# Expert layer with a fixed room of 832 rows for each expert, its weights standing and its rows moving, and attention matmuls in halves

## What is computed

```python
for t in range(S):                                   # attention
    state = f[:, :, t, :, None] * state + np.einsum('bhd,bhe->bhde', k[:, :, t], v[:, :, t])
    y[:, :, t] = np.einsum('bhd,bhde->bhe', q[:, :, t], state)
...
noisy_logits = x @ w_gate + np.log1p(np.exp(x @ w_noise)) * noise
top2 = np.argpartition(-noisy_logits, 2, axis=1)[:, :2]
...
h = np.maximum(x[mask] @ w1[e], 0.0)                 # w1: 384 x 1024, for each of 8 experts
out[mask] += top2_w[mask, k, None] * (h @ w2[e])     # w2: 1024 x 384
...
g = h - np.tanh(h)                                   # h = x @ w_in, 384 x 2048
return g @ w_out                                     # 2048 x 384
```

## Time and profile before

| | |
|---|---|
| runs shown, median | 1233.32 us (1232.97 to 1234.04) |
| the profiled execution, its own time | 1235.88 us |
| its span, first to last instruction | 1234.0 us |
| PE busy | 1121.3 us, 91% of the span |
| DVE, ACT, POOL busy | 482.3, 371.4, 264.9 us |
| chain that ended last | PE 83%, DVE 8%, issue 3% |

### The profile page before, as it was taken

One profiled execution on the slowest core, in us unless ns is written; L12 is line 12 of the kernel. 1 busy time (PEld: TensorE's weight loads), 2 busy tenths in 40 slices (PEclk: granted clock), 3 DMA queues, 4 the chain that ended last, 5 costly groups with the idle time before them and its releaser, 6 DMA issues.

```text
span 1234.0 us, 17874 instructions
## 1 busy us (share of the span) xinstructions
PE 1121.3 (91%) x6761; PEld 1011.8 (82%) x6762; DVE 482.3 (39%) x946; ACT 371.4 (30%) x707; POOL 264.9 (21%) x167
## 2 busy tenths in 40 slices
PE   4999796806999999999999999759999999999999
PEld 3888685805999999989998999649999999999998
DVE  3777574743222222222222222254343433434333
ACT  3444332321222222222222222323233332333322
POOL 1001203064242504224051433032010111100000
PEclk9999787957999999999999999969999999999999
DMA  8213213154323221314141414021020101110000
GB/s 330 70 67 99 94 59 134 48 202 172 141 63 117 96 89 54 132 39 145 42 143 38 147 38 147 31 71 52 1 65 13 52 26 42 37 39 13 21 6 26
DMA packets 34271, 98.71 MB, mean 80 GB/s; under 512 B 4784, under 2 KB 23344, under 8 KB 31152
## 3 DMA queue, kind: packets, MB, share of 16 engines
q0 software_dynamic: 9024, 50.34, 11.9%
q1 hardware_dynamic: 17136, 36.71, 9.0%
q10 hardware_dynamic: 8064, 11.01, 2.4%
HBM read 70.71 MB, written 27.33 MB: 79 GB/s over the span
## 4 chain that ended last, share of the span: by engine, by line
PE 83%; DVE 8%; issue 3%; DMA 2%; another core or an unknown queue 2%; ACT 1%; DVEq 0%; SPq 0%; POOL 0%; ACTq 0%
PE bank L762 18%; PE bank L754 18%; PE bank L852 16%; PE bank L864 16%; PE bank L775 4%; PE bank L650 2%; PE bank L674 2%; PE bank L768 1%; DMA noise_sb<-noise 1%; PE bank L671 1%; DVE kT L938 1%; DVE state L967 1%; PE bank L626 1%; PE bank L658 1%
## 5 line engine op out<-in xcount | busy, mean ns | idle before, releaser
L864 PE MATMUL bank<-slots,g_hi 128*128 128x384 f32 x768 | 196.5, 336 | 0.0
L754 PE MATMUL bank<-slots,x_hi 128*128 128x512 f32 x624 | 166.6, 403 | 2.8 <-issue 1.5
L762 PE MATMUL bank<-slots,h_hi 128*128 128x384 f32 x832 | 159.9, 344 | 2.6 <-DVE h_lo L1229 2.6
L852 PE MATMUL bank<-dx_hi,slots 128*128 128x512 f32 x576 | 152.4, 400 | 1.3 <-DVE dx_lo L1262 1.3
L864 PEld LDWEIGHTS bank<-slots,g_hi 128*128 128x128 f32 x768 | 141.2, 188 | 8.2
L762 PEld LDWEIGHTS bank<-slots,h_hi 128*128 128x128 f32 x832 | 144.8, 190 | 2.9 <-issue 2.9
L754 PEld LDWEIGHTS bank<-slots,x_hi 128*128 128x128 f32 x624 | 114.9, 191 | 26.7 <-issue 4.0
L864 PE MATMUL bank<-slots,g_lo 128*128 128x384 f32 x384 | 129.6, 337 | 0.0
L852 PEld LDWEIGHTS bank<-dx_hi,slots 128*128 128x128 f32 x576 | 106.8, 190 | 19.1 <-issue 1.6
L517 ACT ACTIVATE h_hi<-bank 128x512 fp32r<-128x512 f32 x104 | 56.5, 595 | 203.8 <-PE bank L775 203.8
L1271 DVE TENSOR_TENSOR g_lo<-g,g_hi 128x512 fp32r<-128x512 f32 x96 | 66.5, 692 | 121.2 <-ACT g_hi L574 121.2
(11 more groups left out here) (151 smaller groups left out, 1456.2 us busy)
## 6 DMA issues: line engine op xcount, KB each, us to landing
raw_w<-w_all POOLq DMA_DIRECT2D x20, 1536.0 KB, 7.0
qkv_sb<-qkv SPq DMA_DIRECT2D x24, 576.0 KB, 3.7
xg<-expert_rows SPq DMA_DIRECT2D x53, 192.0 KB, 2.3
expert_outs<-y_sb ACTq DMA_DIRECT2D x52, 192.0 KB, 1.9
f_exp<-f SPq DMA_DIRECT2D x4, 1152.0 KB, 17.8
out<-d_out SPq DMA_DIRECT2D x24, 192.0 KB, 2.0
expert_outs<-zeros SPq DMA_DIRECT2D x7, 192.0 KB
expert_rows<-zeros ACTq DMA_DIRECT2D x4, 192.0 KB, 1.9
```

The lines of the kernel that those rows point to most:

```text
L754: done = mm(ps[:, :], x_part[:, k, :], slots[:, base + at:base + at + BANK], start=n == 0 and k == 0, stop=n == 2 and k == DK - 1)
L762: done = mm(pO[:, 0:D], h_part[:, k, :], slots[:, base + at:base + at + D], start=start and n == 0 and k == 0, stop=stop and n == 2 and k ...
L852: done = mm(pDH[s % 2][:, :], slots[:, at:at + P], x_part[:, b % 2, k, :], start=n == 0 and k == 0, stop=n == 2 and k == DK - 1)
L864: done = mm(pD[j][:, 0:D], g_part[:, s % 2, j * P:(j + 1) * P], slots[:, at:at + D], start=c == 0 and n == 0, stop=c == FC - 1 and n == 2)
```

## The change

1. Every expert has a fixed room of `CAP` = 832 rows in `expert_rows`, and results lie at the same place in `expert_outs`. The table `meta` and `out_row_a/b` go away; a block behind `If(overflowing(...))` on each engine handles rows beyond 832, and does not run with the inputs here.
2. The expert layer takes the form of the dense one: 16 parts (448 and 384 rows of each expert), 8 steps of 128 hidden columns each, all written out. Weights are stationary and rows move on the way up (9 matmuls of 448 or 384 columns); on the way down there are 4 or 3 tiles, each 3 matmuls of 384 columns. Nothing is transposed between them. Copies of results go half to ACT, half to DVE, and SP stores them.
3. The whole room is filled with zeros at the start, by 8 DMAs of 832 rows (10.2 MB together) that ACT issues ahead of its first activation; the first scatter waits for them (`zeroed`).
4. The matmuls with the state, with `am` and of the gate scores are cut into two halves of 64 output rows, twice as many as before.
5. `route_rows` has two operations more; rows of the dense layer are split one step later (`c - 1 in X_STEPS`).

```diff
+PIECES = (448, 384)
+CAP = sum(PIECES)
...
+HALVES = (slice(0, P // 2), slice(P // 2, P))
...
             sp.wait_ge(scattered, 2 * NT * 16)
             sp.wait_ge(early_done, 1)
+            load_rows(0)
+            load_rows(1)
+            for i in range(len(PARTS)):
+                if i + 2 < len(PARTS):
+                    sp.wait_ge(m_xT_ps, M_FIRST[i + 1])
+                    load_rows(i + 2)
+                store_rows(i)
...
+            pool.wait_ge(zeroed, -(-CLEARED // CAP) * 16)
             for g in range(B):
                 scatter(g, g)
...
+            act.wait_ge(zeros_ready, 1)
+            for row in range(0, CLEARED, CAP):
+                some = expert_rows[row:min(row + CAP, CLEARED), :].rearrange("(p j) d -> p j d", p=P // 2)
+                act.dma_start(some, zeros[0:P // 2, :].unsqueeze(1).to_broadcast(list(some.shape))).then_inc(zeroed, 16)
             act.wait_ge(L_zeroed, 1)
             decay_exp(0, f_in[0], 16)
...
+            for s in range(M_STEPS):
+                i, c = divmod(s, FK)
+                m_h_high(s)
+                if i + 1 < len(PARTS) and 1 <= c <= M_TILES[i + 1]:
+                    m_x_high(i + 1, c - 1)
+                if i >= 1 and c == 1:
+                    m_results(i - 1)
+            m_results(len(PARTS) - 1)
...
-                    done = mm(pG[:, D:D + GATES], xT32[:, k * P:(k + 1) * P], wr[:, k, :],
-                              start=k == 0, stop=k == DK - 1)
+                    for half in HALVES:
+                        cols = slice(k * P + half.start, k * P + half.stop)
+                        done = mm(pG[half, D:D + GATES], xT32[:, cols], wr[:, k, :],
+                                  start=k == 0, stop=k == DK - 1)
...
-                    mm(pY[:, c0:c0 + 2 * HD], qT[:, a, :], state[:, a, :, :].rearrange("p c d -> p (c d)"),
-                       start=True, stop=False, skip_group_check=True)
+                    for half in HALVES:
+                        mm(pY[half, c0:c0 + 2 * HD], qT[:, a, half], state[:, a, :, :].rearrange("p c d -> p (c d)"),
+                           start=True, stop=False, skip_group_check=True)
...
+            def m_up_chunk(s):
+                i, c = divmod(s, FK)
+                e, off, n = PARTS[i]
+                if c == 0:
+                    pe.wait_ge(m_xlo, M_FIRST[i + 1])
+                    if off == 0:
+                        pe.wait_ge(w_split, 2 * (e + 1))
+                if s >= 2:
+                    pe.wait_ge(m_hlo, s - 1)
+                for q, (lo, x_part) in enumerate(up_terms):
+                    for k in range(DK):
+                        at = e % 2 * SLOT + lo * PART + k * F + c * P
+                        done = mm(pDH[s % 2][:, 0:n], slots[:, at:at + P], x_part[:, i % 2, k, 0:n],
+                                  start=q == 0 and k == 0, stop=q == 2 and k == DK - 1)
+                done.then_inc(m_up, 1)
+
+            def m_down_chunk(s):
+                i, c = divmod(s, FK)
+                e, off, n = PARTS[i]
+                pe.wait_ge(m_hlo, s + 1)
+                for j in range(M_TILES[i]):
+                    if c == 0 and i >= 1 and j < M_TILES[i - 1]:
+                        pe.wait_ge((m_y_act, m_y_dve)[j % 2], y_done(i - 1, j))
+                    first = part_out(n, j)
+                    for q, (g_part, lo) in enumerate(((g_hi, 0), (g_hi, 1), (g_lo, 0))):
+                        at = e % 2 * SLOT + lo * PART + WCOLS + c * D
+                        done = mm(pD[j][:, 0:D], g_part[:, s % 2, first:first + P], slots[:, at:at + D],
+                                  start=c == 0 and q == 0, stop=c == FK - 1 and q == 2)
...
+            for s in range(M_STEPS):
+                i, c = divmod(s, FK)
+                if i + 1 < len(PARTS) and c < M_TILES[i + 1]:
+                    m_rows(i + 1, c)
+                if s + 2 < M_STEPS:
+                    m_up_chunk(s + 2)
+                m_down_chunk(s)
...
-            chain(vec.tensor_tensor(cmp3[:, :, :], over_tiles(cnt[:, :], NT),
-                                    over_experts(cst[:, C_ROW:C_ROW + NT], NT), ALU.is_gt))
...
-            vec.tensor_copy(meta[:, :], metaf[:, :]).then_inc(meta_ready, 1)
+            chain(vec.tensor_reduce(most[:, :], cnt[:, :], X_AXIS, ALU.max))
+            vec.tensor_scalar(over[:, :], most[:, :], float(CAP), None, ALU.is_gt).then_inc(over_ready, 1)
+            vec.tensor_copy(spare_v[:, :], most[:, :]).then_inc(early_done, 1)
```

More of the change, by code:

```diff
@@ L61, with part_tiles, part_tile, part_out @@
 X_STEPS = (4, 6, 8, 10)
+PARTS = [(e, off, n) for e in range(E) for off, n in zip((0, PIECES[0]), PIECES)]
+M_STEPS = len(PARTS) * FK
+def part_tiles(n):
+    return -(-n // P)
+def part_tile(n, j):
+    return j * P, min(P, n - j * P)
+def part_out(n, j):
+    return min(j * P, n - P)
+M_TILES = [part_tiles(n) for _, _, n in PARTS]
+M_FIRST = [sum(M_TILES[:i]) for i in range(len(PARTS) + 1)]
+def y_done(i, j):
+    before = sum((m + 1 - j % 2) // 2 for m in M_TILES[:i])
+    return before + j // 2 + 1
 C_ID, C_DECAY, C_CAUSAL, C_TRI, C_ONES = 0, P, 2 * P, 3 * P, 4 * P
@@ L513, in _ @@
-            hh = h_hi[:, :, :].rearrange("p a c -> p (a c)")
-            def halves(out_, func, banks, signal):
-                for j, ps in enumerate(banks):
-                    last = nc.scalar.activation(out_[:, j * BANK:(j + 1) * BANK], ps[:, :], func)
-                last.then_inc(signal, 1)
-            def x_high(t):
-                act.wait_ge(xT_ps, t + 1)
-                nc.scalar.activation(xh, pXT[:, 0:D], ACT.Copy).then_inc(xhi_ready, 1)
-            def relu(t):
-                act.wait_ge(h_ps, t + 1)
-                halves(h_sb, ACT.Relu, (pH0, pH1), h_ready)
@@ L547, in _, with m_down_done, m_x_high @@
-            store(act.value_load(meta[0:1, M_LAST:M_LAST + 1], min_val=E - 1, max_val=MAX_TILES - 1))
+            def m_down_done(s):
+                i, c = divmod(s, FK)
+                if c == FK - 1:
+                    act.wait_ge(m_y_ps, M_FIRST[i + 1])
+                else:
+                    act.wait_ge(m_down, s + 1 - i)
+            def m_x_high(i, j):
+                first, rows = part_tile(PARTS[i][2], j)
+                t = M_FIRST[i] + j
+                act.wait_ge(m_xT_ps, t + 1)
+                nc.scalar.activation(dx_hi[:, i % 2, :, first:first + rows],
+                                     pDX[t % 2][:, 0:D].rearrange("p (k c) -> p k c", k=DK)[:, :, 0:rows], ACT.Copy
+                                     ).then_inc(m_xhi, 1)
@@ L549, in _ @@
+            act.wait_ge(m_y_ps, M_FIRST[-1])
             for j in range(2):
@@ L803, in start_of @@
-            def start_of(e):
-                return pe.value_load(meta[0:1, bass.ds(e + M_START, 1)], min_val=1, max_val=MAX_TILES)
-            def more_tiles(start, end, slot):
-                with pe.If(end > start):
-                    with pe.Fori(start, end) as t:
-                        tile(t, slot * SLOT, slot * SLOT)
-            def expert(e, slot, start, end):
-                pe.wait_ge(w_split, e * 2 + 2)
-                tile(start, slot * SLOT, (1 - slot) * SLOT)
-                more_tiles(start + 1, end, slot)
@@ L829, in _, with m_rows @@
-            expert_down(last_tile, SLOT)
-            d_terms = ((0, dx_hi), (1, dx_hi), (0, dx_lo))
+            up_terms = ((0, dx_hi), (1, dx_hi), (0, dx_lo))
+            def m_rows(i, j):
+                first, rows = part_tile(PARTS[i][2], j)
+                t = M_FIRST[i] + j
+                if j == 0:
+                    pe.wait_ge(xg_in[i % 2], 16 * sum(1 + (n % P > 0) for _, _, n in PARTS[i % 2:i + 1:2]))
+                if t >= 2:
+                    pe.wait_ge(m_xlo, t - 1)
+                for k in range(DK):
+                    done = nc.tensor.transpose(pDX[t % 2][:, k * P:k * P + rows],
+                                               xg[0:rows, i % 2, j, k * P:(k + 1) * P], ident[0:rows, 0:rows])
+                done.then_inc(m_xT_ps, 1)
```

452 lines of the change are left out of this document (215 added, 237 removed).

## The result

| | before | after |
|---|---|---|
| median of 7 runs each | 1233.32 us (1232.97 to 1238.13) | 1237.63 us (1236.61 to 1238.28) |
| span of the profiled execution | 1234.0 us | 1235.2 us |

The account below looks back on a forecast made before the run. TensorE was taken to bound the expert and dense layers, chains on other engines the gaps. Start +3, attention -8, way to experts -3.8, experts -36.6, experts to dense +1 gave -44.4 us: 1189 us, range 1173 to 1209.

Parts of the forecast that it names:

- The start: Up to PE's chunk 0: zeros in busy DMA engines and 8 issues ahead of ACT's first activation cost +3 us.
- the zeros hold up the start: Rival at the start: ACT's issues wait for queue room, about +20 us in place of +3, 1206 us; chance 0.15.
- upper bound of 28 us: At the start: delay if all loads waited for the 10.2 MB of zeros, moved at 364 GB/s.
- The 7 us: Landing of noise at the start: half as late again with three queues in turn instead of two; sum 4 us higher.
- Attention: Attention stage: halved pY and gate matmuls save 0.8 us in 8 plain chunks, 0.2 in 16 others; -8 us in all.
- halves gain nothing: Rival in attention: PE's drain at each change of shape eats the halves' gain, 1197 us; chance 0.08.
- halves dear: Rival in attention: each half costs as much as a whole matmul, +76 us, 1273 us; chance 0.04.
- Attention to experts: From attention's end to the first expert matmul: 41.2 in place of 45 us, -3.8, DVE's split done in time.
- Experts: Expert layer: steps of 3.93 and 3.15 us without transposes of h, 470 us against 506.6, -36.6 us.
- waits between parts: Rival in the expert layer: 15 changes of part cost 2 us each, +30, 1219 us; chance 0.03.
- Experts to dense: Between expert and dense layers: two copies on ACT and three stores on SP cost +1 us on 23.3.
- dense: Dense layer: unchanged at 414 us, 0 us, since PE there has no wait for rows.

Follow-up runs that it names:

- fill_pool_at_once: Changed kernel with all 8 fills issued by POOL right behind its own two loads, without waiting for the first loads: 1189.95 us, 0.9852 of the kernel before.
- fill_pool: Changed kernel with all 8 fills issued by POOL once gate weights and noise have landed, not by ACT: 1191.67 us, 0.9859 of the kernel before.
- group 4: Runs on one chip: spread and late_split again, and late_split with halves undone; 1194.40, 1190.61 and 1200.60 us against 1232.88 for the kernel before.
- before_halves: Kernel before with only the halves of the attention and gate matmuls added: 1218.99 us, 0.9891 of the kernel before.
- late_split_b: Repeat of late_split, beside spread_b on one chip: 1190.61 us, 0.9661 of the kernel before.
- spread_b: Repeat of spread, beside late_split_b on one chip: 1194.40 us, 0.9685 of the kernel before.
- late_split: Spread, with DVE waiting for the last scatter before it splits expert 0's weights: 1191.34 us, 0.9668 of the kernel before.
- spread: Changed kernel with the 8 fills issued by POOL one by one, each behind the pY of another attention chunk: 1179.34 us, 0.9761 of the kernel before.
- group 2: Runs on one chip: both kernels again, and spread with and without the halves; the kernel before took 1207.66 us there.

## Why the prediction was wrong, step by step

**The start (+3, measured +44.6) is the step that failed**, and within it the sentence that 8 issues ahead of ACT's first activation cost "no more than the 0.97 us of one of POOL's issues", 8 us in all. A POOL issue of 128 rows says nothing of ACT's fifth issue of 832 pieces: on POOL eight such fills take 0.8 us each even one behind the other, on ACT only the first two are that cheap. The rival *the zeros hold up the start* named the right mechanism (the issues wait for room in a queue), at 0.15 and with +20 us, and its upper bound of 28 us was no bound: it took 364 GB/s from a window in which loads ran, while the fills alone move 195. 10.2 MB at 195 GB/s are 52 us, which is the hold of 52.31 us; that the two agree so closely is partly chance, since the loads ran in between and fills were still under way when ACT was free. The evidence "against" the rival, that other issues take well under 1 us beside the same traffic, was of issues with little queued ahead of them. The first two fills behaved just so.

What the step says of the load of noise was right. Issued at 4.14 us, noise landed 17.0 later, at 21.1, where before it was there at 17.9; fill_pool_at_once started PE's chunk 0 at 19.8. That is +2 to +3. But the step stopped at chunk 0. Had ACT not been held, the loads of q/k/v for the next chunks would have come late, as in fill_pool and fill_pool_at_once, which gained 17 and 19 us on their chip and not some 40; no term of the sum had this. The 7 us that came out of the round of the queues as the Trainium skill tells it ("DMA: Bandwidth & Descriptors", Queues, rings and completion order) were too many: the trace has 17.0 us in place of 14.6, not half as much again.

**Attention (-8, measured -10.7)**: right for the plain chunks, whose gain was put too low; that the sum came so close is in part luck. A plain chunk of the changed kernel (timeline of PE):

```profile
87.11 0.53 PE L684 MATMUL bank<-wr,xT 128*64 128x16 f32 x12
87.48 0.65 PE L716 MATMUL bank<-qkv_sb,ks 128*64 128x48 f32 x16
...
88.64 0.39 PE L730 MATMUL bank<-state,qT 128*64 128x96 f32 x4
...
89.08 0.35 PE L730 MATMUL bank<-state,qT 128*64 128x96 f32 x4
...
89.26 0.39 PE L734 MATMUL bank<-qkv_sb,am 128*64 128x48 f32 x8
...
89.48 0.35 PE L730 MATMUL bank<-state,qT 128*64 128x96 f32 x4
...
90.37 0.66 PE L692 MATMUL bank<-cst,qs 128*128 128x128 f32 x4
```

pY takes 90.37 - 88.64 = 1.73 us where 2.1 was forecast and 2.6 stood in the earlier trace rows: 48 halves at 0.036 us on average (counted as in the forecast, each float32 matmul twice), those with 96 columns at (89.26 - 89.08) / 4 = 0.045 and those with 48 at (89.48 - 89.26) / 8 = 0.028, where I had taken 0.056 and 0.038. The gate scores take 0.37 us (forecast 0.46, before 0.77). A plain chunk falls from 8.0 to 6.7 us, by 1.3 where 0.8 was forecast. Why two halves cost less than one whole was not asked of the traces. The seven stretches from kT to kT of the first sequence fall from 56.7 to 49.4 us, 7.4 of the 10.7. The sixteen behind them fall by 2.3 (162.1 to 159.8), but one of them alone, the 16th, which runs partly at 1.2 GHz in the kernel before only, by 4.0; and two that do so in the changed kernel only, the 9th and the 15th, rise by 1.4 and 1.2. So the -0.2 us forecast for each chunk with other work beside it is not shown here; group 4, without its two long stretches, gives 0.16. The drain of TensorE at a change of tiling mode, by which the Trainium skill's "TensorEngine Tiling (Array Packing)", Key Properties, speaks against this edit, shows as no loss here: with one change more per chunk the chunk got 1.3 us shorter, where the two groups by themselves account for 1.3. The rivals *halves gain nothing* and *halves dear* fall with before_halves.

**Attention to experts (-3.8, measured +0.6)**: here the sentence failed that DVE's split of expert 0 "now starts earlier and is done by then". It does start earlier, and that is the trouble. In the kernel before, the 18 operations for `meta` kept it off until POOL's scatter was through the earlier trace rows (timeline of DVE):

```profile
274.49 6.62 DVE L1202 TENSOR_TENSOR slots<-raw_w,slots 128x3072 fp32r<-128x3072 f32 x2
```

In the changed kernel, it falls into the scatter (timeline of POOL and DVE):

```profile
293.42 0.97 POOL L367 DMA_INDIRECT expert_rows<-x_all,row_b  x1 [0.30 <-issue]
293.62 6.62 DVE L1232 TENSOR_TENSOR slots<-raw_w,slots 128x3072 fp32r<-128x3072 f32 x2
294.70 3.12 POOL L367 DMA_INDIRECT expert_rows<-x_all,row_a  x1 [0.30 <-issue]
298.12 2.96 POOL L367 DMA_INDIRECT expert_rows<-x_all,row_b  x1 [0.30 <-issue]
301.39 0.97 POOL L367 DMA_INDIRECT expert_rows<-x_all,row_a  x1 [0.30 <-issue]
...
312.86 0.97 POOL L367 DMA_INDIRECT expert_rows<-x_all,row_b  x1 [0.30 <-issue]
```

Two of POOL's issues take 3.12 and 2.96 us in place of 0.97 exactly while the split runs, and everything behind them is 4.1 us later, the rows of part 0 among it. The stage is 4.4 us longer than the 41.2 forecast; the rest are terms that cancel, a scatter that starts 0.3 us behind the end of attention and not 1.1 ahead of it (+1.4), and loads and first tiles 1.3 us quicker than summed. The Trainium skill, "SBUF — State Buffer", Who interferes with whom, names a likely reason: DVE and GpSimd share a pair of ports, and a DVE instruction with two inputs in SBUF, as this one has, contends with a GpSimd instruction that reads SBUF. The trace agrees: the two splits (3.35 us each) end at 296.97 and 300.24, and the slow issues at 297.82 and 301.08, each 0.85 us behind the end of a split, which is little less than an undisturbed issue takes. The same section infers that an instruction of this kind leaves alone the descriptors that GpSimd makes for a DMA; for these indirect DMAs, whose row numbers lie in `row_a` and `row_b` in SBUF, the measurement says otherwise. That it is the reading of these numbers that waits is not shown. It was the rule to weigh in the forecast. In late_split_b the split waits for the scatter, and no issue is slow (timeline of POOL and DVE):

```profile
265.35 0.97 POOL L371 DMA_INDIRECT expert_rows<-x_all,row_b  x1 [0.30 <-issue]
267.95 6.63 DVE L1233 TENSOR_TENSOR slots<-raw_w,slots 128x3072 fp32r<-128x3072 f32 x2 [17.61 <-DMA expert_rows<-x_all,row_b]
```

Its scatter takes 29.5 us from first to last issue in place of 33.7, and the stage 42.0 us, near the 41.2 of the forecast. In spread_b, on the same chip, two issues take 3.11 and 2.97 us, and the stage 45.9.

**Experts (-36.6, measured -34.3)**: right. Two neighbouring steps with 448 rows and two with 384 in the changed kernel, without transposes:

```profile
342.71 1.40 PE L828 MATMUL bank<-dx_hi,slots 128*128 128x448 f32 x6
...
346.65 1.40 PE L828 MATMUL bank<-dx_hi,slots 128*128 128x448 f32 x6
...
787.25 1.20 PE L828 MATMUL bank<-dx_hi,slots 128*128 128x384 f32 x6
...
790.37 1.20 PE L828 MATMUL bank<-dx_hi,slots 128*128 128x384 f32 x6
```

3.94 and 3.12 us, forecast 3.93 and 3.15: 452 us for all 128, where 453 was forecast. The remaining 20.5 us of the stage were put at 17 (13 for transposes of rows, 3 for the start, 1 for changes of part). One expert's 16 steps take 59.0 us (342.71 to the same step at 401.71), 2.5 more than 16 plain ones, in the steps that transpose 7 tiles of rows; so it is the transposes that were put too low. Nothing stands between up and down, PE is busy 472.22 of 472.30 us, and the 15 changes of part cost nothing that shows, which settles the rival *waits between parts*. **Experts to dense** came to +0.8 us (+1) and **dense** to +0.2 (0).

So the sum without the hold on ACT, without disturbed loads and with the split out of the scatter's way, was sound: late_split_b takes 1190.61 us where before takes 1232.88 (-42.3 us; the forecast was -44.4), with every part of the change in it. It is the fastest version of those that ran on its chip, 3.4% below the kernel before (spread_b, the next, lies 3.8 us above it, with an overlapping interval); late_split, on another chip where before takes much the same time (1231.12 us), gave 0.9668.

## What to carry over

A DMA issue is not free just because its landing is not waited for: a large transfer in many pieces, issued ahead of an engine's own work, can hold that engine for nearly as long as the transfer moves, as ACT was here for 52 us. Issue such a fill from where it holds nobody (POOL, here), in small portions behind events of the main loop, and keep it off the stretch in which the loads for the critical path run: with the fills moved to POOL in one go the changed kernel was 17 us faster than the kernel before, with the fills spread out 28 and 38 us (on two chips). And when a chain of small operations is removed, look at what it kept apart: here it kept a long DVE operation out of POOL's scatter. A bandwidth for a bound must come from a row of the same direction and shape of transfer.

## What had not been expected of the hardware

- DMA engines at 88 to 89% busy moved only 195 GB/s when fills from SBUF to HBM ran alone, and some 400 with loads beside them. Pieces of 4992 bytes in place of 1536 changed it to 204, so the piece's size is not the limit; what is was not tried (all fills read the same 64 partitions).
- An issue on ACT took 1 us for the first two fills and 4 to 14 us from the third; a third of the pieces halved the hold. POOL's own issues of the same fills took 0.8 us each in fill_pool, all eight in a row, and 0.8 to 1.0 in spread.
- Chips that run the dense and the expert stage alike to 0.1% differ by 8% in attention (227.1 and 208.2 us). In the trace of before on the first chip DVE waits 9.22 us, put down to `remote`, in a chunk beside a scatter, and such a chunk takes 18.2 us; on the chip of group 2 it takes 11.6. What it waits for is open.
- Leaving the fills out was not tried: without them some rows of the rooms are never written.
